# Seven block products in place of eight in the first matmul of each layer of a gated scan with two feed-forward layers

## What is computed

```
x [2, 6080, 256], f_logit [2, 6080, 256], lower_bound [256]
f = lower_bound + (1 - lower_bound) * sigmoid(f_logit)
h[t] = f[t] * h[t-1] + (1 - f[t]) * x[t]          # along the 6080 steps of each batch
x1 = h as 12160 tokens x 256
layer 1:  u = x1 @ w_in1 (256 x 2048);  g = u - tanh(u);         y1 = g @ w_out1 (2048 x 256)
layer 2:  u = y1 @ w_in2 (256 x 2048);  g = max(0.01 * u, u);    out = g @ w_out2 (2048 x 256)
```

## Time and profile before

| | |
|---|---|
| Median of 3 runs (lowest to highest) | 2087.35 us (2086.33 to 2088.47) |
| The profiled execution: span from first to last instruction | 2085.9 us |
| TensorE matmul busy | 2077.4 us, 9234 instructions (18 of them on zeros) |
| VectorE busy | 1165.1 us, 1837 instructions |
| ScalarE busy | 958.0 us, 1760 instructions |
| GpSimd busy | 0.7 us, 5 instructions |
| Mean granted TensorE clock | 0.999 |
| DMA | 46.05 MB, mean 22 GB/s |

### The profile page before, as it was taken

One profiled execution on the slowest core, in us unless ns is written; L12 is line 12 of the kernel. 1 busy time (PEld: TensorE's weight loads), 2 busy tenths in 40 slices (PEclk: granted clock), 3 DMA queues, 4 the chain that ended last, 5 costly groups with the idle time before them and its releaser, 6 DMA issues.

```text
span 2085.9 us, 26437 instructions
## 1 busy us (share of the span) xinstructions
PE 2077.4 (100%) x9234; PEld 1728.6 (83%) x9234; DVE 1165.1 (56%) x1837; ACT 958.0 (46%) x1760; POOL 0.7 (0%) x5
## 2 busy tenths in 40 slices
PE   9999999999999999999999999999999999999999
PEld 7888888888888888888888888888888888888887
DVE  7755555555555555555555555555555555555444
ACT  6544444444444444444444444444444444444444
POOL 0000000000000000000000000000000000000000
PEclk9999999999999999999999999999999999999999
DMA  5100000000000000000000000000000000000000
GB/s 176 62 8 21 31 8 23 10 20 30 4 26 10 20 30 1 29 10 20 30 0 30 10 20 30 0 30 10 20 30 0 30 10 20 30 0 10 10 0 21
DMA packets 24409, 46.05 MB, mean 22 GB/s; under 512 B 1857, under 2 KB 2625, under 8 KB 24385
## 3 DMA queue, kind: packets, MB, share of 16 engines
q1 hardware_dynamic: 24384, 45.75, 6.4%
HBM read 33.29 MB, written 12.45 MB: 22 GB/s over the span
## 4 chain that ended last, share of the span: by engine, by line
PE 99%; DMA 0%; DVE 0%; SPq 0%; ACT 0%; issue 0%
PE h_ps L229 17%; PE h_ps L230 17%; PE h_ps L231 17%; PE y_ps L242 17%; PE y_ps L243 17%; PE y_ps L241 17%; DMA w_stage<-w_in 0%; DVE w_lo L462 0%; DVE y_lo L513 0%; DVE state L499 0%; DVE gate L642 0%; ACT w_hi L327 0%; DVE drive L483 0%; SPq L191 0%; SPq L190 0%; SPq L188 0%
## 5 line engine op out<-in xcount | busy, mean ns | idle before, releaser
L524 DVE TENSOR_TENSOR g_full<-h_ps,bent 128x512 f32<-128x512 f32 (+1 forms) x768 | 526.2, 685 | 908.8 <-ACT bent L356 516.2
L242 PE MATMUL y_ps<-g_lo,w_hi 128*128 128x512 f32 (+1 forms) x1536 | 594.1, 387 | 0.0
L243 PE MATMUL y_ps<-g_hi,w_lo 128*128 128x512 f32 (+1 forms) x1536 | 594.0, 387 | 0.0
L241 PE MATMUL y_ps<-g_hi,w_hi 128*128 128x512 f32 (+1 forms) x1536 | 594.0, 387 | 0.0
L531 DVE TENSOR_TENSOR g_lo<-g_full,g_hi 128x512 fp32r<-128x512 f32 (+1 forms) x768 | 518.6, 675 | 0.1
L356 ACT ACTIVATE bent<-h_ps 128x512 f32<-128x512 f32 (+1 forms) x384 | 227.9, 594 | 588.3 <-PE h_ps L231 588.3
L354 ACT ACTIVATE bent<-h_ps 128x512 f32<-128x512 f32 (+1 forms) x384 | 228.0, 594 | 524.8 <-PE h_ps L231 524.3
L365 ACT CAST g_hi<-g_full 128x512 fp32r<-128x512 f32 (+1 forms) x768 | 467.4, 609 | 0.7 <-DVE g_full L524 0.7
L241 PEld LDWEIGHTS y_ps<-g_hi,w_hi 128*128 128x128 f32 x1536 | 288.4, 188 | 57.5
L242 PEld LDWEIGHTS y_ps<-g_lo,w_hi 128*128 128x128 f32 x1536 | 288.4, 188 | 57.5
L243 PEld LDWEIGHTS y_ps<-g_hi,w_lo 128*128 128x128 f32 x1536 | 288.4, 188 | 57.3
(11 more groups left out here) (30 smaller groups left out, 501.2 us busy)
## 6 DMA issues: line engine op xcount, KB each, us to landing
logit<-f_logit SPq DMA_DIRECT2D x23, 512.0 KB, 3.7
drive<-x SPq DMA_DIRECT2D x23, 512.0 KB, 4.6
out<-y_out SPq DMA_DIRECT2D x22, 512.0 KB, 2.8
w_stage<-w_in SPq DMA_DIRECT2D x16, 256.0 KB, 5.2
w_stage<-w_out SPq DMA_DIRECT2D x16, 256.0 KB, 2.8
out<-gate SPq DMA_DIRECT2D x2, 256.0 KB, 2.0
logit<-f_logit SPq DMA_DIRECT2D x2, 192.0 KB, 2.7
drive<-x SPq DMA_DIRECT2D x2, 192.0 KB, 3.3
```

Of the source, the lines that this page charges most:

```text
L241: nc.tensor.matmul(bank, w_hi[m][:, c, k, :], g_hi[:, b, :W], start=c == 0, stop=False)
L242: nc.tensor.matmul(bank, w_hi[m][:, c, k, :], g_lo[:, b, :W], start=False, stop=False)
L243: mm = nc.tensor.matmul(bank, w_lo[m][:, c, k, :], g_hi[:, b, :W], start=False, stop=c == NF - 1)
L524: nc.vector.tensor_tensor(g_full[:, c % GB, :W], h_ps[:, c % HB, :W], bent[:, c % 2, :W], ALU.subtract if layer == 1 else ALU.max).then_in ...
```

## The change

**The block products.** The first matmul of each layer is taken as a 2 x 2 by 2 x 2 block product: two halves of the contraction (k), two chunks of the hidden dimension (f), and two blocks of tokens (b), one from each batch. Seven products of sums of blocks replace the eight of the plain form. A *tile* s is now 512 tokens of both batches (the last of a layer 448), 12 tiles for layer 1 (s = 0 to 11), then 12 for layer 2 (s = 12, `SWITCH`, to 23, `END`). A *slot* is one pair of hidden chunks (a group g of 8) of one tile: 7 x 3 matmuls of the first product and 8 x 3 of the second (for the slot before). Sums that several blocks share are built in one PSUM bank (`x_ps`, the *chain*: four products one on top of the other), and ScalarE copies the state of the bank to SBUF (`copy_chain`) after each of the first three, before the next may be added. VectorE adds the products of `p_ps` and `q_ps` to these copies (`add_c11`, `add_c22`, `add_c12`). The last state of the chain is the fourth block, C21.

**The order of the layers.** All tokens go through layer 1, whose result is stored to DRAM (`y1`) and loaded again for layer 2 (`raw`). Only the weights of one layer lie in SBUF: those of layer 2 replace them during s = 11 (`LAST`) and the start of s = 12.

**The operands.** Each tile's x blocks take four sums (`sums13`, `sums2`, `sums4` on VectorE) and seven high and low parts (`x_round` on ScalarE, `x_split` on VectorE), where the kernel before had four of each for as many tokens. The sums of the weights are made on GpSimd (`sum_weights`), and so are the low parts of the weights (`wi_split` of 896 columns, `wo_split` of 512).

**The low parts of g.** Of the four blocks of a slot, those of C11 and C12 are made by VectorE and those of C22 and C21 by GpSimd. In layer 2 VectorE makes C11, C22 and C12 of g in one instruction each, without ScalarE.

**The start.** 60 matmuls on zeros in place of 18.

The diff, cut to its core (of the removed lines only the constants stand here, since the functions before are printed above; left out too are the DMA lists, the TensorE loop over slots, and helpers of one instruction, which are described here):

```diff
@@ -28,18 +5,31 @@
-LAG = 3
-HB = 4
-GB = 4
-WB = 6
 LEAK = 0.01
-WARM = 18
+WARM = 60
+GROUPS = 8
+TILES = 12
...
+W22, W11, W12, S1, S2, S3, S4 = range(7)
+X11, T2, X21, T3, T1, T4, X22 = range(7)
+C11, C22, C21, C12 = range(4)
+BLOCK_OF = ((0, 0), (1, 1), (1, 0), (0, 1))
...
+    def width(s):
+        return W_LAST if isinstance(s, int) and s % TILES == LAST else BANK
+    y1 = nc.dram_tensor("y1", (KD, P, N), F32, kind="Internal").ap()
...
+            def product(bank, g, w, i, W, start, stop):
+                hi, lo = wi_hi[:, g, w, :], wi_lo[:, g, w, :]
+                nc.tensor.matmul(bank, hi, x_hi[:, i, :W], start=start, stop=False, skip_group_check=True)
+                nc.tensor.matmul(bank, hi, x_lo[:, i, :W], start=False, stop=False, skip_group_check=True)
+                return nc.tensor.matmul(bank, lo, x_hi[:, i, :W], start=False, stop=stop, skip_group_check=True)
...
+                if isinstance(s, int) and s in (0, SWITCH):
+                    pe.wait_ge(wi_ready, (0 if s == 0 else GROUPS) + g + 1)
+                if g == 0:
+                    pe.wait_ge(x_ready, 7 * s + 1)
+                if not (first and g < 2):
+                    pe.wait_ge(full_ready, 4 * (q - 2) + 3)
+                product(chain, g, W11, X11, W, True, False).then_inc(chain_done, 1)
+                y(C11, 0)
+                y(C11, 1)
+                y(C22, 0)
+                if g == 0:
+                    pe.wait_ge(x_ready, 7 * s + 2)
+                pe.wait_ge(chain_copied, 3 * q + 1)
+                product(chain, g, S2, T2, W, False, False).then_inc(chain_done, 1)
+                if g == 0:
+                    pe.wait_ge(x_ready, 7 * s + 3)
+                if not (first and g == 0):
+                    pe.wait_ge(c11_ready, q)
+                product(p_bank, g, W12, X21, W, True, True).then_inc(p_done, 1)
+                y(C22, 1)
+                y(C21, 0)
+                if g == 0:
+                    pe.wait_ge(x_ready, 7 * s + 4)
+                pe.wait_ge(chain_copied, 3 * q + 2)
+                product(chain, g, S3, T3, W, False, False).then_inc(chain_done, 1)
+                if g == 0:
+                    pe.wait_ge(x_ready, 7 * s + 5)
+                if not (first and g == 0):
+                    pe.wait_ge(c12_ready, q)
+                product(q_bank, g, S1, T1, W, True, False).then_inc(q_done, 1)
+                y(C21, 1)
+                y(C12, 0)
+                if g == 0:
+                    pe.wait_ge(x_ready, 7 * s + 6)
+                pe.wait_ge(chain_copied, 3 * q + 3)
+                product(chain, g, W22, T4, W, False, True).then_inc(chain_done, 1)
+                if g == 0:
+                    pe.wait_ge(x_ready, 7 * s + 7)
+                pe.wait_ge(c22_ready, q + 1)
+                product(q_bank, g, S4, X22, W, False, True).then_inc(q_done, 1)
+                y(C12, 1)
...
+            def wo_round(n):
+                act.wait_ge(wo_in[n % 2], 16 * (n // 2 + 1))
+                if n >= GROUPS:
+                    act.wait_ge(g_used, 4 * (8 * LAST + n - GROUPS) + 4)
                 nc.scalar.copy(
...
+            def copy_chain(q, par, i, W):
+                act.wait_ge(chain_done, 4 * q + i + 1)
+                nc.scalar.copy(part[:, par, i, :W], x_ps[:, par, :W]).then_inc(chain_copied, 1)
...
+            def drain(s, b, k):
+                W = width(s)
+                act.wait_ge(g_used, 4 * (8 * s + 7) + (3 if b == 0 else 4))
+                if k == 0 and b == 0 and not (isinstance(s, int) and s == 0):
+                    act.wait_ge(y_stored, 32 * s)
+                nc.scalar.copy(y_out[:, b, k, :W], y_ps[:, k, b, :W]).then_inc(y_drained, 1)
+            def slot(s, g, layer, scans, preps):
+                q = 8 * s + g
+                W = width(s)
+                par = g % 2
+                first = isinstance(s, int) and s == 0
+                if g == 1 and not first:
+                    drain(s - 1, 1, 0)
+                copy_chain(q, par, 0, W)
+                if g == 1 and not first:
+                    drain(s - 1, 1, 1)
+                if not (first and g == 0):
+                    if g == 0:
+                        round_g(s - 1, 7, C12, width(s - 1))
+                    else:
+                        round_g(s, g - 1, C12, W)
+                if g == 0 and not first:
+                    x_round(s, T1)
+                    x_round(s, T4)
+                if g == 7 and preps:
+                    x_round(s + 1, X11)
+                if scans and g in (1, 2, 3, 4):
+                    squash(s + 1, g - 1)
+                copy_chain(q, par, 1, W)
+                if g == 0 and not first:
+                    x_round(s, X22)
+                if g == 7 and preps:
+                    x_round(s + 1, T2)
+                    x_round(s + 1, X21)
                 if layer == 1:
+                    bend(s, g, C11, W)
+                copy_chain(q, par, 2, W)
+                round_g(s, g, C11, W)
+                if first:
+                    wo_round(g)
+                    if g + 1 < GROUPS:
+                        wi_round(g + 1)
+                if isinstance(s, int) and s == LAST and g >= 1:
+                    wi_round(GROUPS + g - 1)
+                if isinstance(s, int) and s == LAST and g >= 2:
+                    wo_round(GROUPS + g - 2)
...
+                if g == 7 and preps:
+                    x_round(s + 1, T3)
+                if layer == 1:
+                    bend(s, g, C22, W)
+                    bend(s, g, C21, W)
                 else:
+                    leak(s, g, W)
+                round_g(s, g, C22, W)
+                round_g(s, g, C21, W)
+                if layer == 1:
+                    bend(s, g, C12, W)
+                if g == 0 and not first:
+                    drain(s - 1, 0, 0)
+                    drain(s - 1, 0, 1)
...
+            def add_c11(q, par, W):
+                dve.wait_ge(p_done, q + 1)
+                dve.wait_ge(chain_copied, 3 * q + 1)
+                nc.vector.tensor_tensor(
+                    part[:, par, 0, :W], p_ps[:, :W], part[:, par, 0, :W], ALU.add
+                ).then_inc(c11_ready, 1)
...
+            def slot(s, g, layer, prev, scans, preps):
+                q = 8 * s + g
+                W = width(s)
+                par = g % 2
+                first = isinstance(s, int) and s == 0
+                if not (first and g == 0):
+                    W_before = width(s - 1) if g == 0 else W
+                    make_g(q - 1, 1 - par, C12, W_before, prev if g == 0 else layer)
+                    if scans and g in (1, 2, 3, 4):
+                        forget_gate(s + 1, g - 1)
+                    split_g(q - 1, 1 - par, C12, W_before)
+                if g == 0 and not first:
+                    x_split(s, T1, 4)
+                    x_split(s, T4, 5)
+                if g == 7 and preps:
+                    x_split(s + 1, X11, 0)
+                if scans and g in (1, 2, 3, 4):
+                    drive_term(s + 1, g - 1)
+                add_c11(q, par, W)
+                if g == 0 and not first:
+                    x_split(s, X22, 6)
+                if g == 7 and preps:
+                    x_split(s + 1, T2, 1)
+                    x_split(s + 1, X21, 2)
+                if scans and g in (1, 2, 3, 4):
+                    scan(s + 1, g - 1)
+                if preps and g == 5:
+                    if scans:
+                        keep_states(s + 1)
+                    sums13(s + 1, 1 if scans else 2)
+                if preps and g == 6:
+                    sums2(s + 1)
+                make_g(q, par, C11, W, layer)
+                add_c22(q, par, W)
+                split_g(q, par, C11, W)
+                if g == 7 and preps:
+                    x_split(s + 1, T3, 3)
+                if preps and g == 6:
+                    sums4(s + 1)
+                make_g(q, par, C22, W, layer)
+                make_g(q, par, C21, W, layer)
+                add_c12(q, par, W)
...
+            def sum_weights(n):
+                st = wi_stage[:, n % 2, :, :]
+                pool.wait_ge(wi_in[n % 2], 16 * (n // 2 + 1))
+                nc.gpsimd.tensor_tensor(st[:, 4, :], st[:, 0, :], st[:, 1, :], ALU.add).then_inc(s1_ready, 1)
+                nc.gpsimd.tensor_tensor(st[:, 6, :], st[:, 2, :], st[:, 0, :], ALU.subtract)
+                pool.wait_ge(s1_ready, n + 1)
+                nc.gpsimd.tensor_tensor(st[:, 5, :], st[:, 4, :], st[:, 2, :], ALU.subtract).then_inc(s2_ready, 1)
+                pool.wait_ge(s2_ready, n + 1)
+                nc.gpsimd.tensor_tensor(st[:, 7, :], st[:, 3, :], st[:, 5, :], ALU.subtract).then_inc(sums_w_ready, 1)
+            def wi_split(n):
+                g = n % GROUPS
+                pool.wait_ge(wi_hi_ready, n + 1)
+                nc.gpsimd.tensor_tensor(
+                    wi_lo[:, g, :, :], wi_stage[:, n % 2, 1:8, :], wi_hi[:, g, :, :].bitcast(F32), ALU.subtract
```

(76 more changed lines are left out.)

864 lines of the change are left out of this document (474 added, 390 removed).

## The result

The changed kernel takes 2093.01 us (median of 10 runs, 2090.89 to 2096.36) against 2088.11 (10 runs, 2086.0 to 2089.2): ratio 1.0025, 95% interval 1.0017 to 1.0034, slower by a quarter of a per cent. The forecast was 2022 us, with a range of 1975 to 2085. The profiled execution has a span of 2091.1 us, 70.5 more than the forecast sum of 2020.6.

What follows compares the result with a forecast made beforehand. TensorE was taken as the bound, by number and pace of matmuls: 1938.2 + 23.7 + 18 + 22 + 10 + 5 + 3.65 = 2020.6 us of span, the median 1.45 above: 2022 us, range 1975 to 2085.

Steps and rivals of the forecast that it cites:

- part 1: Matmuls: 45 a slot in place of 48, at 0.2266 us for 512 columns; 1938.2 against 2067.4 us, -129 us.
- the likeliest case: The whole kernel: the forecast itself, 2022 us with its own range 1995 to 2055; chance 0.60.
- Part 2: Ordinary slot: without GpSimd's part the other engines keep TensorE fed, 10.2 us a slot; VectorE and ScalarE not full.
- Part 3: GpSimd's price: 1.28 us per 512-column instruction, no stall; 5 us in all if it and VectorE exclude each other.
- Part 4: Emptying y_ps: first y of slot 1 waits for the drain, 1.26 us in layer 1, 0.67 in layer 2; +22 us.
- Part 5: The start, +9 us (23.7 lost where 14.9 was), and tile 0's slots waiting on GpSimd's weight work, +18 us.
- sign of being wrong: Clock: the forecast would be wrong if the clock left 1.00 in the pauses of TensorE; no size given.
- Part 6: Second layer's weights: around s = 11 GpSimd's extra work makes C22's split late eight times; +10 us.
- rival 2: GpSimd becomes the bound: slower than before from 1.95 us per instruction, 2145 us at 2.1; chance 0.12.
- The 0.86 for "faster": The whole kernel: chance 0.86 of being faster than before, against 0.02 for same and 0.12 for slower.

Runs made afterwards that it cites:

- the first three changes: Changed kernel with carry allocated last, earlier copies out of y_ps and earlier rounding of weights together: missed the 2028 us sum of the gains by 7 us.
- The last run: Changed kernel with carry last, earlier y_ps copies, earlier weight rounding, low parts of g and of weights on VectorE: 9.9 us gained on 2023, 3.6% less than before.

## Why the prediction was wrong, point by point

- **The step that failed is part 1.** It took 0.2266 us a matmul from the kernel before and put it on other buffers. The count was right (45 a slot, 8640), the pace was not: 0.2323, 46 of the 70 us. Rows 4 and 5 were taken as a property of the instruction, and were one of the instruction and of where the tiles lie. The diff showed a tile of 16 bytes ahead of `g_hi`; I didn't read the order of allocation as part of the change. This is shown by undoing it (2056 us, faster than before) and by doing the same to the kernel before (2148). The 2056 us lie in the range, just past the likeliest case's own 1995 to 2055. By what path a 16-byte shift slows even the matmuls of x is open.
- **Part 2 held.** Undisturbed slots have no wait of TensorE at all, with copies, additions and tanh in between.
- **Part 3 held in its price**: GpSimd's 512-column subtractions have a median of 1.30 us, 1.28 was taken; the mean is 1.46 with the waits for VectorE. Exclusion was given as open and is real. In undisturbed slots it costs nothing. In layer 1 slots 2 and 4 lose 0.2 us each, which no run puts down to a cause.
- **Part 4 held**: 1.33 and 0.80 us were measured, 1.26 and 0.67 forecast, some 24 us in all against 22. Moving the copies gave back 20.
- **Part 5 was too small**: 36.6 us to slot 1 (28.5), then 13.95 us a slot (13.2 with the 18 us over six slots). The third scan accounts for a part: it took 3.02 us where the first two took 1.22, and GpSimd's `wi_split` of slot 0 ran from 14.67 to 16.74 beside it:

```profile
14.80 3.02 DVE L644 TENSOR_TENSOR_SCAN raw<-y_out,full 128x512 f32<-128x512 f32 x1
```

  The four sums of weights, 128 columns each, also took 2.3 us and more a slot. TensorE started nothing from 17.4 to 27.0 us meanwhile, and its granted clock was 0.63 from 20 to 25 us and 0.50, the level of 1.2 GHz, from 25 to 30. Nine matmuls from 27.5 us on followed 0.427 us apart, some 2 us in all for which the forecast had no term; it named the clock only as a sign of being wrong.
- **Part 6 was too small by 8 us**: at the start of tile 12 GpSimd had `wi_lo` (from 1070.54) and `wo_lo` (to 1074.34) ahead of C22's low part, which then waited 1.16 for its high part, and TensorE stood 3.65 us:

```profile
1076.69 0.74 PE L292 MATMUL y_ps<-g_hi,wo_hi 128*128 128x448 f32 x1 [3.65 <-POOL g_lo L859]
```

- **The rivals.** The sign came out as rival 2's, but not by its mechanism: GpSimd took 1.30 us, far from the 1.95 from which it decides. No rival was about the pace of a matmul. The 0.86 for "faster" rested on the row of the pace, for which I gave no range.

## What to carry to other kernels

A matmul's distance to the next is a quantity to measure for each kernel from start to start; busy shares hide it. Where a change moves the operands of the bounding engine, read the order of allocation with it, and keep small tiles behind the large ones. Give GpSimd two-operand work only where VectorE's own two-operand SBUF work has room for the whole length of it; and on a pair of banks that is used again at once, put the copy out of it early in its engine's list.

## What the runs showed of the hardware that was not expected

- TensorE, moving operands of 512 float32r columns in the kernel before: 0.2267 us a step where they start on a multiple of 256 bytes or more behind tiles of whole 2 KB; 0.229 on average at 64 bytes, 0.2333 at 16. Only these shifts were tried.
- Uneven steps of up to 0.236 us come in aligned kernels too, for some ten matmuls behind a wait, and then settle at 0.2267 (run of the first three changes together, tile 0, from 37.99 us to 40.1). With the shift they don't settle.
- At 448 columns the step doesn't go by the shift: in undisturbed slots of the last tile it was 0.204 us (9.18 us / 45) with g shifted by 16 bytes and 0.2067 (9.30 / 45) aligned, but 0.2027 (9.12 / 45) in one aligned run, that of the first three changes. The last run had 0.2027 in a slot of tile 11 and 0.2067 in the last tile. Not explained.
- Beside GpSimd, a VectorE subtraction with two SBUF operands took up to 2.57 us in the changed kernel (2.62 over all runs) in place of 0.68, the additions with an operand in PSUM never more than 0.694.
